# In each attention step, the scalar engine's exponential is issued ahead of the ring's evictions

## The chip, the cores and the metric

The kernel runs on one core of a Trainium2 chip. The time is device time from start to end of one launch, in microseconds (us). The core's engines each run their own instruction list in order and meet only through semaphores: TensorE (PE, with its weight loads shown as PEld), VectorE (DVE), ScalarE (ACT), GpSimd (POOL) and SyncE (SP), which issues the transfers.

## What is computed

Three layers in a row: attention, a mixture of experts, and a gated MLP. The change touches the attention alone, which is this (batch 4, 8 heads, 576 tokens, head size 64):

```python
scores = q @ k.T / sqrt(64)
thresh = max(scores, axis=-1) - tau
scores = where(scores >= thresh, scores, -1e9)
attn = exp(scores - max(scores, axis=-1))
attn = attn / (sum(attn, axis=-1) + 1e-09)
out = attn @ v
```

Its output feeds a router (logits, argmax, a scan over the tokens of a batch, ranks per expert), then the experts and the last layer.

## The kernel before, in words

**Units and steps.** Two heads make a pair; there are 16 pairs. A pair has 9 units (`W = 9`) of 128 rows of scores by 576 columns, the last of them packed from the two heads' last 64 rows. So there are 144 units, and the program is a list of numbered steps, one for each unit and some after them. I write w0 to w8 for the place of a step in its pair, S(w) for the score product of unit w, and "of the pair before" where a step of one pair handles work of the last.

**What each engine does in step n.**

- PE first computes the scores of unit n+1 into one of three score buffers in PSUM (`ps_s`, L556 and L557). It waits there until the mask of unit n-2 is done, since that frees the buffer. Then it fills the items of step n.
- DVE takes the row maximum of unit n (L802), normalises the pv items of step n-1 (L841), masks unit n-1 (L816: keep what is above the floor, times the exponential, with the row sum), and makes the floor of unit n (L807). In w1 it also sums and inverts a whole pair's row sums (L823, L830).
- ACT takes the exponential of unit n (L467; it waits for the row maximum of unit n) and evicts the items of step n that are not DVE's (L510; each waits for its fill). In w2 and w3 it also scales half of the next pair's q (L463). POOL splits q and k into high and low parts for the pair after.

**The ring.** All transposes and products after the scores go through a ring of two PSUM banks, `ps_ring`. Item number i may be filled only when item i-2 has been taken out. The items of a pair, in order of filling, with the step in which they stand:

| step | items filled by PE (line) | taken out by |
|---|---|---|
| w3 to w8, then w0 and w1 of the next pair | main 0 to 7: four transposes of one unit's probabilities (L604) | ACT |
| w2 of the next pair | tails and last: what is left of the transposes (L610, L616) | ACT |
| w4 of the next pair, ahead of its main item | sums and rest (L620 to L626) | ACT |
| w5, w7 of the next pair, w0, w2 of the one after | pv 0 to 3: 20 products of transposed probabilities and v (L635), last in their step | DVE |

So w2 holds tails, last, pv 3, and pv 3 can start only when tails has been evicted; in w4, main 1 can start only when sums has been evicted. In pairs 5 to 7, 9 to 11 and 13 to 15 some steps hold a router item more (logits, rows, spread), and w1 of pairs 8 and 12 holds two. The router item rows 3 stands in w6 behind main 3, and can be filled only when DVE has taken pv 0 of step w5 out. The scan over a batch's tokens (L898) stands on DVE at the end of w5 of pairs 7, 11 and 15.

Nothing plans the order: it is what the step loops of the functions say. Here they are, with the lines that the change touches:

Of the kernel before, what the change touches and what calls it, by code (L numbers as in the profile page):

```python
# [52 lines left out]
def rows(t):  # L53
    return P if t < FULL else TAIL
# [10 lines left out]
UNITS = ALL_PAIRS * W  # L65
# [18 lines left out]
def after_batch(b, at):  # L84

    return PAIRS * W * (b + 1) + at
# [60 lines left out]
def taken_from_ring(kind, i, of):  # L147

    return taken(filled(kind, i, of))
# [7 lines left out]
def unit_of(n):  # L157

    return divmod(n, W)


def attention(nc, ctx, io, route):
# [127 lines left out]
    def q_head(h, part):  # L290

        return q_split[0][part, (S + TAIL) * h:(S + TAIL) * h + S]

    def scores(n):
        return ps_s[:, n % SLOTS_S, :, 0:HALF]
# [162 lines left out]
    def scalar_steps(act, steps, row_banks=None):  # L458

        def scale_q(pair, h):  # L460

            act.wait_ge(q_loaded, 32 * pair + 32)
            nc.scalar.mul(q_in[:, h, :], q_in[:, h, :], float(DH) ** -0.5).then_inc(q_scaled, 1)  # L463

        def exp_scores(n):
            act.wait_ge(maxed, n + 1)
            nc.scalar.activation(expd[:, n % SLOTS_S, :].rearrange("p (a c) -> p a c", a=2), scores(n), ACT.Exp,  # L467
                                 bias=max_tau[:, n % 4, 0:1]).then_inc(exped, 1)

        def evacuate(no, item):  # L470

            kind, i, of = item
            act.wait_ge(turned, no + 1)
            bank = ps_r[:, no % 2, :]
            pt = probs_t[of % 2]
            if kind == "main":
                t, h = divmod(i, 2)
                out, src = pt[:, FULL * h:FULL * h + FULL, P * t:P * t + P], bank.rearrange("p (c q) -> p c q", c=FULL)
            elif kind == "tails":
                out, src = pt[:, W - 1, 0:FULL * P], bank  # L480
            elif kind == "last":
                out = pt[:, 0:2 * FULL, FULL * P:S].rearrange("p (h c) q -> p c h q", h=2)
                src = bank.rearrange("p (c h q) -> p c h q", c=FULL, h=2)
            elif kind == "sums":
                if of >= 2:

                    act.wait_ge(dve_took, taken_from_ring("pv", PIECES - 1, of - 2))
                out, src = pt[:, W, 0:FULL * P], bank
            elif kind == "rest":
                nc.scalar.copy(pt[0:DH, W - 1:W + 1, FULL * P:S], bank[0:DH, 0:2 * P].rearrange("p (a q) -> p a q", a=2)[:, :, 0:TAIL])  # L490
                out, src = pt[DH:P, W - 1:W + 1, FULL * P:S], bank[DH:P, 0:2 * P].rearrange("p (a q) -> p a q", a=2)[:, :, TAIL:P]
            elif kind == "logits":
                r = rows(i)
                out, src = logits[0:r, i, :], bank[0:r, 0:E + 1]
            elif kind == "early":
                nc.scalar.copy(logits[0:TAIL, FULL, :], bank[0:TAIL, FULL * (E + 1):QT * (E + 1)])
                out, src = logits[:, 0:FULL, :], bank[:, 0:FULL * (E + 1)].rearrange("p (t e) -> p t e", t=FULL)
            elif kind == "rows":
                if i == 0 and of > 0:

                    act.wait_ge(rows_stored, 32 * of)
                r = rows(i)
                out, src = x_rows[0:r, i, :], bank[0:r, 0:D]
            elif kind == "spread":
                cols = FULL * P if i == 0 else TAIL
                out, src = code_r[:, FULL * P * i:FULL * P * i + cols], bank[0:E, 0:cols]
            else:
                nc.scalar.copy(onehot_t[0:TAIL, FULL, :], bank[0:TAIL, FULL * E:QT * E])
                out, src = onehot_t[:, 0:FULL, :], bank[:, 0:FULL * E].rearrange("p (t e) -> p t e", t=FULL)
            nc.scalar.copy(out, src).then_inc(evacuated, 1)  # L510

        def last_rows(i):

            act.wait_ge(rows_turned, i + 1)
            if i == 0:

                act.wait_ge(rows_stored, 32 * (B - 1))
            r = rows(i)
            nc.scalar.copy(x_rows[0:r, i, :], row_banks[i][0:r, :]).then_inc(rows_out, 1)

        def exp_logits(b):
            act.wait_ge(shift_done, b + 1)
            nc.scalar.activation(exp_l[:], shifted[:], ACT.Exp).then_inc(exp_done, 1)

        if steps.start == 0:
            for h in range(2):
                act.wait_ge(q_loaded if h else q_first, 32)
                nc.scalar.mul(q_in[:, h, :], q_in[:, h, :], float(DH) ** -0.5).then_inc(first_scaled, 1)
                act.wait_ge(first_scaled, h + 1)
                nc.scalar.copy(q_head(h, slice(0, P)), q_in[:, h, :]).then_inc(first_cast, 1)  # L530

        for n in steps:
            pair, w = unit_of(n)
            for k, item in enumerate(STEPS[n]):
                if item[0] not in BY_DVE:
                    evacuate(FIRST_OF_STEP[n] + k, item)
            if n < UNITS:
                exp_scores(n)
            for h in range(2):
                if w == SCALE_AT[h] and pair + 1 < ALL_PAIRS:  # L540
                    scale_q(pair + 1, h)
            for b in range(B):
                if n == after_batch(b, ARGMAX_AT + 1 if b < B - 1 else LAST_ARGMAX_AT):
                    exp_logits(b)
            for i in range(QT):
                if n == after_batch(B - 1, LAST_ROWS_AT[i]):
                    last_rows(i)

    @block.scalar
    def _(act):  # L550
        scalar_steps(act, range(MAIN_STEPS))
# [468 lines left out]
    def _(dve):  # L1020
# [4 lines left out]
    left = range(MAIN_STEPS, len(STEPS))  # L1025
    return Ending(
        sync=lambda sp: store_rows(sp, B - 1), scalar=lambda act, row_banks: scalar_steps(act, left, row_banks),
        tensor=lambda pe, row_banks: tensor_steps(pe, left, row_banks), vector=lambda dve: vector_steps(dve, left),
        probs=lambda dve: vector_steps(dve, range(len(STEPS), len(STEPS) + 1)), rows_stored=rows_stored, slots_known=slots_known,
# [747 lines left out]
```

## Time and profile before

| | |
|---|---|
| median of three runs | 981.18 us (978.01 to 984.55) |
| profiled execution | 986.12 us, of which the span is 984.3 us |
| attention | from the start to about 376 us of the span |
| PE busy | 907.7 us, 92% of the span |
| DVE busy | 552.4 us, 56% |
| ACT busy | 416.1 us, 42% |
| POOL busy | 381.5 us, 39% |

The profiled execution is 4.9 us above the median. PE is the busiest engine over the whole span. In the attention stage the other engines are busy too: the page's slices show PE at 8 or 9 tenths, DVE at 7 and ACT at 6 through the first eleven of 40 slices. How to read a time line: start, length, engine, line, what it writes from what it reads, how many instructions are merged, and in brackets how long the engine stood idle before it and which instruction ended that. A length includes an end that overlaps the next instruction: a copy of 0.59 us on ACT is followed by the next instruction 0.48 us after its start.

### The profile page before, as it was taken

What the parts mean: (1) busy time and instruction counts of PE and PEld (TensorE: products, weight loads), DVE (VectorE), ACT (ScalarE), POOL (GpSimd) and SP (SyncE); (2) the same over time, 40 slices, a digit from 0 to 9 for tenths busy, and PEclk for the clock granted to TensorE, in tenths of its full rate; (3) what the DMA queues carried; (4) which work ended last, traced back from release to release, by engine and by line L of the source; (5) the groups of instructions that cost most, each with busy time, mean ns of one, the idle gap of its engine ahead of it and who ended that gap; (6) DMA issues with size and microseconds to landing.
All of it is one profiled execution on the core that took longest, in us unless ns stands there. A gap on an engine that the chain in (4) does not pass through costs nothing.

```text
span 984.3 us, 16278 instructions
## 1 busy us (share of the span) xinstructions
PE 907.7 (92%) x6007; PEld 766.9 (78%) x6007; DVE 552.4 (56%) x1206; ACT 416.1 (42%) x794; POOL 381.5 (39%) x347
## 2 busy tenths in 40 slices
PE   6899998999889993999999999999879999999996
PEld 5777887788778782788888888788669788798885
DVE  6777777777777726705846578460034435344351
ACT  4766666666666623233333333333323122131220
POOL 4344435644473133345655556554204013040100
PEclk8999999999999986899999999999979999999998
DMA  5323322232232016423656376430030020200101
GB/s 147 74 61 87 83 74 61 62 110 62 72 109 63 13 49 232 157 89 122 214 162 196 129 220 200 154 101 19 0 109 1 1 97 1 83 14 1 49 1 49
DMA packets 47709, 86.82 MB, mean 88 GB/s; under 512 B 8076, under 2 KB 16396, under 8 KB 47632
## 3 DMA queue, kind: packets, MB, share of 16 engines
q1 hardware_dynamic: 43632, 76.32, 25.9%
q0 software_dynamic: 4000, 9.45, 3.0%
q8 instruction: 51, 0.84, 0.4%
q14 instruction: 26, 0.21, 0.1%
HBM read 73.42 MB, written 15.99 MB: 91 GB/s over the span
## 4 chain that ended last, share of the span: by engine, by line
PE 51%; DVE 6%; DMA 4%; issue 1%; ACT 1%; POOL 0%; DVEq 0%; POOLq 0%
PE ps_h L1357 4%; PE ps_h L1359 4%; PE ps_h L1358 4%; PE ps_y L1376 4%; PE ps_y L1378 4%; PE ps_y L1377 4%; PE ps_a L1639 4%; PE ps_a L1640 4%; PE ps_a L1641 4%; PE ps_v L1639 3%; DMA w_raw<-in_w 3%; PE ps_v L1641 2%; PE ps_v L1640 2%; PE ps_r L1639 2%; PE ps_r L1640 2%; PE ps_r L1641 2%
## 5 line engine op out<-in xcount | busy, mean ns | idle before, releaser
L816 DVE SCALAR_TENSOR_TENSOR probs<-ps_s,floor,expd 128x576 f32<-128x576 f32 x144 | 117.1, 813 | 62.0 <-ACT expd L467 61.6
L510 ACT COPY probs_t<-ps_ring 128x512 f32<-128x512 f32 (+1 forms) x192 | 105.9, 560 | 102.5 <-PE ps_ring L604 93.4
L1289 DVE CAST w_high<-w_raw 128x1024 fp32r<-128x1024 f32 (+1 forms) x63 | 66.8, 1076 | 103.6 <-PE ps_h L1359 52.1
L556 PE MATMUL ps_s<-k_high,q_split 128*128 128x288 f32 x336 | 107.0, 336 | 15.1 <-DVE probs L816 11.1
L467 ACT ACTIVATE expd<-ps_s,max_tau 128x576 f32<-128x576 f32 x144 | 108.0, 750 | 4.8 <-DVE max_tau L802 4.7
L802 DVE TENSOR_REDUCE max_tau<-ps_s 128x1 f32<-128x576 f32 x144 | 106.8, 742 | 0.0
L635 PE MATMUL ps_ring<-probs_t,v_pair 128*64 128x144 f32 x1280 | 94.8, 296 | 3.6 <-ACT probs_t L510 3.6
L556 PEld LDWEIGHTS ps_s<-k_high,q_split 128*128 128x128 f32 x336 | 64.6, 192 | 36.4 <-DVE probs L816 25.3
L557 PE MATMUL ps_s<-k_low,q_split 128*128 128x288 f32 x336 | 92.6, 298 | 0.0
L635 PEld LDWEIGHTS ps_ring<-probs_t,v_pair 128*64 128x64 f32 x1280 | 78.2, 140 | 14.7 <-ACT probs_t L510 7.1
L604 PE MATMUL ps_ring<-ident,probs 128*128 128x128 f32 x512 | 80.0, 279 | 8.0 <-ACT probs_t L510 8.0
L1516 POOL TENSOR_TENSOR rstd<-var_eps,exponent 128x1 f32<-128x1 f32 (+1 forms) x20 | 17.0, 849 | 180.7 <-DVE var_eps L1578 180.7
L1357 PE MATMUL ps_h<-w_high,x_slot_t_high 128*128 x200 | 82.8, 414 | 4.4 <-POOL x_slot_t_low L1179 2.4
L1376 PE MATMUL ps_y<-w_high,hidden_t_high 128*128 128x512 f32 x200 | 80.9, 405 | 2.3 <-DVE w_low L1297 1.9
L1297 DVE TENSOR_TENSOR w_low<-w_raw,w_high 128x1024 fp32r<-128x1024 f32 x66 | 80.8, 1246 | 0.0
L1359 PE MATMUL ps_h<-w_high,x_slot_t_low 128*128 x200 | 79.7, 398 | 0.0
L1358 PE MATMUL ps_h<-w_low,x_slot_t_high 128*128 x200 | 79.4, 397 | 0.0
L1378 PE MATMUL ps_y<-w_high,hidden_t_low 128*128 128x512 f32 x200 | 78.4, 392 | 0.0
L1377 PE MATMUL ps_y<-w_low,hidden_t_high 128*128 128x512 f32 x200 | 77.9, 390 | 0.0
L1191 POOL DMA_INDIRECT y_rows_dram<-scratch,ids x25 | 32.6, 1303 | 113.6 <-ACT scratch L1240 113.6
L604 PEld LDWEIGHTS ps_ring<-ident,probs 128*128 128x128 f32 x512 | 61.3, 142 | 12.2 <-ACT probs_t L510 11.4
L1229 ACT ACTIVATE scratch<-ps_h 128x512 f32<-128x512 f32 x50 | 29.9, 599 | 90.3 <-PE ps_h L1359 84.9
(238 smaller groups left out, 2058.5 us busy)
## 6 DMA issues: line engine op xcount, KB each, us to landing
w_raw<-in_w SPq DMA_DIRECT2D x64, 512.0 KB
k_in<-in_k SPq DMA_DIRECT2D x30, 288.0 KB, 4.2
q_in<-in_q SPq DMA_DIRECT2D x30, 288.0 KB, 4.2
v_pair<-in_v SPq DMA_DIRECT2D x16, 256.0 KB, 2.7
x_rows_dram<-scratch SPq DMA_DIRECT2D x4, 1024.0 KB, 4.6
out<-scratch SPq DMA_DIRECT2D x4, 1024.0 KB, 4.3
scratch<-in_dense SPq DMA_DIRECT2D x8, 384.0 KB, 6.1
scratch<-y_rows_dram SPq DMA_DIRECT2D x3, 1024.0 KB, 5.5
```

The costliest lines, as they stand in the source:

```text
L467: nc.scalar.activation(expd[:, n % SLOTS_S, :].rearrange("p (a c) -> p a c", a=2), scores(n), ACT.Exp, bias=max_tau[:, n % 4, 0:1]).then_i ...
L556: nc.tensor.matmul(out, lhs, k_high[par][:, h, cols], start=first, stop=False)
L604: last = nc.tensor.transpose(bank[:, P * c:P * c + P], src[:, at + P * c:at + P * c + P], ident[:])
L635: last = nc.tensor.matmul(bank[DH * h:DH * h + DH, 0:PIECE], v[:, c, DH * h:DH * h + DH], pt[:, chunk, cols], start=(c == 0), stop=(c == Q ...
L802: nc.vector.tensor_reduce(max_tau[:, n % 4, 0:1], scores(n), AX_XY, ALU.max, negate=True).then_inc(maxed, 1)
L816: nc.vector.scalar_tensor_tensor(out=row_of(pair, w).rearrange("p (a c) -> p a c", a=2), in0=scores(n), scalar=floor[:, n % 4:n % 4 + 1], ...
L1357: nc.tensor.matmul(ps_h[:, half, :], x_slot_t[0][:, c, :], high[:, cols], start=(c == 0), stop=False)
L1358: nc.tensor.matmul(ps_h[:, half, :], x_slot_t[0][:, c, :], low[:, cols], start=False, stop=False)
L1359: last = nc.tensor.matmul(ps_h[:, half, :], x_slot_t[1][:, c, :], high[:, cols], start=False, stop=(c == DC - 1))
L1376: nc.tensor.matmul(ps_y[:], hidden_t[0][:, c, :], high[:, cols], start=(c == 0), stop=False)
L1377: nc.tensor.matmul(ps_y[:], hidden_t[0][:, c, :], low[:, cols], start=False, stop=False)
L1378: last = nc.tensor.matmul(ps_y[:], hidden_t[1][:, c, :], high[:, cols], start=False, stop=(c == FC - 1))
```

## The change

In every step ACT now issues the exponential ahead of the evictions of the same step. No instruction is added or removed, none changes its form, and only ACT's list is reordered.

```diff
         for n in steps:
             pair, w = unit_of(n)
+            if n < UNITS:
+                exp_scores(n)
             for k, item in enumerate(STEPS[n]):
                 if item[0] not in BY_DVE:
                     evacuate(FIRST_OF_STEP[n] + k, item)
-            if n < UNITS:
-                exp_scores(n)
             for h in range(2):
                 if w == SCALE_AT[h] and pair + 1 < ALL_PAIRS:
                     scale_q(pair + 1, h)
```

ACT, steps w2, w3 and w4 of pair 2, before. `turned` is the count of filled ring items, `maxed` that of row maxima. The two copies at the top are tails and last, the third main 0, then sums, rest in two parts, and main 1.

```order
L510 COPY probs_t<-ps_ring 128x512 [waits turned]
L510 COPY probs_t<-ps_ring 128x4x2x64 [waits turned]
L467 ACTIVATE expd<-ps_s,max_tau 128x576 [waits maxed]
L463 ACTIVATE q_in<-q_in 128x576 [waits q_loaded]
L510 COPY probs_t<-ps_ring 128x4x128 [waits turned]
L467 ACTIVATE expd<-ps_s,max_tau 128x576 [waits maxed]
L463 ACTIVATE q_in<-q_in 128x576 [waits q_loaded]
L510 COPY probs_t<-ps_ring 128x512 [waits turned]
L490 COPY probs_t<-ps_ring 64x2x64 [waits turned]
L510 COPY probs_t<-ps_ring 64x2x64
L510 COPY probs_t<-ps_ring 128x4x128 [waits turned]
L467 ACTIVATE expd<-ps_s,max_tau 128x576 [waits maxed]
```

The same three steps with the change:

```order
L467 ACTIVATE expd<-ps_s,max_tau 128x576 [waits maxed]
L510 COPY probs_t<-ps_ring 128x512 [waits turned]
L510 COPY probs_t<-ps_ring 128x4x2x64 [waits turned]
L463 ACTIVATE q_in<-q_in 128x576 [waits q_loaded]
L467 ACTIVATE expd<-ps_s,max_tau 128x576 [waits maxed]
L510 COPY probs_t<-ps_ring 128x4x128 [waits turned]
L463 ACTIVATE q_in<-q_in 128x576 [waits q_loaded]
L467 ACTIVATE expd<-ps_s,max_tau 128x576 [waits maxed]
L510 COPY probs_t<-ps_ring 128x512 [waits turned]
L490 COPY probs_t<-ps_ring 64x2x64 [waits turned]
L510 COPY probs_t<-ps_ring 64x2x64
L510 COPY probs_t<-ps_ring 128x4x128 [waits turned]
```

Each exponential has moved up past its own step's copies: past tails and last in w2, past main 0 in w3, and past four copies in w4. The scaling of q stays where it was.

ACT at the end of w4 and in w5 and w6 of pair 2, before (main 1, exponential of w4, main 2, exponential of w5, main 3, exponential of w6):

```order
59 L510 COPY probs_t0<-ps_ring 128x4x128 [waits turned]
60 L467 ACTIVATE expd<-ps_s,max_tau 128x576 [waits maxed]
61 L510 COPY probs_t0<-ps_ring 128x4x128 [waits turned]
62 L467 ACTIVATE expd<-ps_s,max_tau 128x576 [waits maxed]
63 L510 COPY probs_t0<-ps_ring 128x4x128 [waits turned]
64 L467 ACTIVATE expd<-ps_s,max_tau 128x576 [waits maxed]
```

and with the change (main 1, exponential of w5, main 2, exponential of w6, main 3):

```order
60 L510 COPY probs_t0<-ps_ring 128x4x128 [waits turned]
61 L467 ACTIVATE expd<-ps_s,max_tau 128x576 [waits maxed]
62 L510 COPY probs_t0<-ps_ring 128x4x128 [waits turned]
63 L467 ACTIVATE expd<-ps_s,max_tau 128x576 [waits maxed]
64 L510 COPY probs_t0<-ps_ring 128x4x128 [waits turned]
```

The exponential of w4 is gone from between main 1 and main 2, since it now stands ahead of sums; otherwise copies and exponentials alternate as before, each exponential one copy earlier.

## Rows read from the trace of the kernel before

**Rows 1.** Waits, 16 to 345 us: who waited for whom, us, times, longest

```profile
ACT probs_t L510 <- PE ps_ring L604: 91.5, 93, 1.6
DVE probs L816 <- ACT expd L467: 60.4, 67, 2.6
```

**Rows 2.** Time line of PE, pairs 3 and 4, without router items

```profile
79.00 1.45 PE L635 MATMUL ps_ring<-probs_t,v_pair 128*64 128x144 f32 x20
...
81.97 0.40 PE L556 MATMUL ps_s<-k_high,q_split 128*128 128x288 f32 x1 [0.36 <-DVE probs L816]
...
83.81 1.45 PE L635 MATMUL ps_ring<-probs_t,v_pair 128*64 128x144 f32 x20
...
86.40 0.40 PE L556 MATMUL ps_s<-k_high,q_split 128*128 128x288 f32 x1
...
87.56 1.45 PE L635 MATMUL ps_ring<-probs_t,v_pair 128*64 128x144 f32 x20
...
92.20 1.45 PE L635 MATMUL ps_ring<-probs_t,v_pair 128*64 128x144 f32 x20 [0.24 <-ACT probs_t L510]
...
97.18 0.66 PE L604 MATMUL ps_ring<-ident,probs 128*128 128x128 f32 x4 [0.67 <-ACT probs_t L510]
```

**Rows 3.** Time line of ACT in the same stretch, w2 to w4

```profile
91.56 1.07 ACT L510 COPY probs_t<-ps_ring 128x512 f32<-128x512 f32 x2
...
95.33 0.75 ACT L467 ACTIVATE expd<-ps_s,max_tau 128x576 f32<-128x576 f32 x1
95.97 0.68 ACT L463 ACTIVATE q_in<-q_in 128x576 f32<-128x576 f32 x1
96.54 0.59 ACT L510 COPY probs_t<-ps_ring 128x512 f32<-128x512 f32 x1
```

**Rows 4.** Time line of DVE in the same stretch

```profile
79.41 0.82 DVE L816 SCALAR_TENSOR_TENSOR probs<-ps_s,floor,expd 128x576 f32<-128x576 f32 x1 [1.47 <-ACT expd L467]
...
85.31 0.31 DVE L841 TENSOR_TENSOR x_t<-ps_ring,probs_t 128x144 f32<-128x144 f32 x1 [0.84 <-PE ps_ring L635]
85.53 0.81 DVE L816 SCALAR_TENSOR_TENSOR probs<-ps_s,floor,expd 128x576 f32<-128x576 f32 x1
...
89.42 0.81 DVE L816 SCALAR_TENSOR_TENSOR probs<-ps_s,floor,expd 128x576 f32<-128x576 f32 x1
...
90.55 0.70 DVE L802 TENSOR_REDUCE max_tau<-ps_s 128x1 f32<-128x576 f32 x1
```

**Rows 5.** Time line of DVE, the first units and the mask of unit 3

```profile
10.84 0.76 DVE L802 TENSOR_REDUCE max_tau<-ps_s 128x1 f32<-128x576 f32 x1
...
13.88 0.81 DVE L816 SCALAR_TENSOR_TENSOR probs<-ps_s,floor,expd 128x576 f32<-128x576 f32 x1
...
15.34 0.81 DVE L816 SCALAR_TENSOR_TENSOR probs<-ps_s,floor,expd 128x576 f32<-128x576 f32 x1
...
19.51 0.82 DVE L816 SCALAR_TENSOR_TENSOR probs<-ps_s,floor,expd 128x576 f32<-128x576 f32 x1 [2.61 <-ACT expd L467]
```

**Rows 6.** Time line of ACT, the first exponentials

```profile
11.63 1.60 ACT L467 ACTIVATE expd<-ps_s,max_tau 128x576 f32<-128x576 f32 x2 [2.84 <-DVE max_tau L802]
```

**Rows 7.** Time line of PE, the first pv product (pair 1, w5)

```profile
39.54 1.45 PE L635 MATMUL ps_ring<-probs_t,v_pair 128*64 128x144 f32 x20
```

**Rows 8.** Windows: us, busy PE, PEld, DVE, ACT, POOL, PEclk, DMA share, GB/s

```profile
22.00:26.00 4.00, 3.92 (x19) 3.81 (x20) 2.91 (x9) 2.12 (x4) 1.98 (x1) 0.57 0.37 72
```

**Rows 9.** Time line of PE, w5 to w7 of pair 7

```profile
162.24 1.45 PE L635 MATMUL ps_ring<-probs_t,v_pair 128*64 128x144 f32 x20
...
166.22 0.66 PE L660 MATMUL ps_ring<-ident,x_t 128*128 128x128 f32 x4 [1.38 <-DVE scratch L841]
...
168.81 1.45 PE L635 MATMUL ps_ring<-probs_t,v_pair 128*64 128x144 f32 x20
```

**Rows 10.** Time line of DVE, end of w4 and w5 of pair 7

```profile
162.64 0.82 DVE L816 SCALAR_TENSOR_TENSOR probs<-ps_s,floor,expd 128x576 f32<-128x576 f32 x1 [1.47 <-ACT expd L467]
...
163.45 1.85 DVE L898 TENSOR_TENSOR_SCAN scratch<-scratch 8x576 f32<-8x576 f32 x1
```

## The prediction

> **What bounds the kernel now.** I read the waits first. ACT waits 91.5 us for transposes in the ring, and DVE waits 60.4 us for the exponential before its masks [rows 1]. So ACT sits waiting for a ring item while the exponential that DVE needs is queued behind that item's copy. Whether this costs anything is a question for PE, which is the busiest engine. So I went to the time lines of one plain pair (without router items), and looked at which of PE's starts has a wait in front of it. I use the four pv products as marks, since each is followed by fixed work. From pv 0 to pv 1 it is 4.81 us, from pv 1 to pv 2 3.75, from pv 2 to pv 3 4.64 [rows 2]. PE stands still at three kinds of places: at S(w8), for a mask; at pv 3, for the copy of tails; at main 1, for the copy of sums [rows 2].
>
> **The shortest chain behind a pv product.** DVE takes a pv item in order, so it holds up the next mask. Where DVE was idle already, the item is taken 1.50 us after the product's start (83.81 to 85.31), the mask starts 0.22 later (85.53), and the score product that needs its buffer 0.87 after that (86.40) [rows 2, 4]. That is 2.59 us, and no order on ACT shortens it. The stretch from pv 1 to pv 2 is on this chain now (83.81 to 86.40 is 2.59), so it stays at 3.75.
>
> **Term A, S(w8): faster.** S(w8) needs the mask of w5, which DVE reaches late, because the mask of w4 before it waited 1.47 us for its exponential [rows 4]. That exponential stood behind the copies of sums, rest (two) and main 1. Now it stands ahead of all four, and DVE is back on the shortest chain: pv 0 + 2.59 to S(w8), and 1.84 more to pv 1 (81.97 to 83.81) [rows 2], 4.43 instead of 4.81. It saves 0.38 us where w6 has no router item: pairs 1 to 4, 8 and 12. Six times, 2.3 us. In the others PE's router work fills the gap already.
>
> **Term B, pv 3: slower.** This is what the order takes back. The copy of tails, which pv 3 needs, now stands behind the exponential of w2, and so behind the row maximum of w2, which comes after pv 2 was taken, a mask, and the summing of the pair's rows. The chain: pv 2 to its taking 1.50, 0.22 to the mask, 1.13 from that mask to the maximum of w2 (89.42 to 90.55) [rows 4], 0.79 from a maximum's start to the exponential (10.84 to 11.63) [rows 5, 6], 0.64 until the next ACT instruction (95.33 to 95.97), and 0.64 from a copy's start to the fill that waits for it (91.56 to 92.20) [rows 2, 3]. Sum 4.92, against 4.64 now: 0.28 lost. It bites where w1 has no router item: pairs 2 to 5, 9 and 13. Six times, minus 1.7 us. Its bounds are 0, if PE is late there for a reason of its own, and 1.0 each, if DVE comes to that maximum one more mask (0.73 from 13.88 to the next unit's maximum, half of 1.46 [rows 5]) later than this chain has it.
>
> **Term C, main 1: nothing.** Main 1 waits for the copy of sums. Before it, ACT does main 0's copy, an exponential and a scaling; now the copy, the scaling and the next exponential: the same two instructions, 95.33 to 96.54, 1.21 us, then 0.64 to main 1 [rows 2, 3]. The stall of 0.67 stays.
>
> **Term D, w6 of pairs 7, 11 and 15: faster.** There the scan follows the mask of w4, and rows 3 may only be filled when pv 0 has been taken, after the scan. The mask of w4 again waited 1.47 us, the scan started at 163.45 and took 1.85, and PE stood 1.38 us at rows 3 [rows 9, 10]. With the change the exponential of w4 goes 2.4 us earlier (it starts one exponential, 0.64, ahead of the copy of sums, instead of behind it by 0.64 for the fill of main 1, about as much until main 1's copy, and 0.48 for that copy; 91.56 holds two copies in 1.07, so one costs 0.48 [rows 3]), so the mask starts near 160.2, the scan near 161.0 (0.81 later, as in rows 10), the maximum of w6 at about 162.9, and DVE is free at 163.5, before pv 0 can be taken (162.24 + 1.50 = 163.74). So the 1.38 goes, and the late mask for S(w8) as in term A, 0.38: 1.8 us. I count 1.8, 1.8 and, in pair 15, whose scan is half a us shorter, 1.3: 4.9 us. Bounds: 0 if something else in that step is late too, 5.4 if all of 1.8 comes three times.
>
> **Term E, the start: faster.** Up to the first pv product PE mostly waits for masks. The exponential of unit 3 waited for a transfer of q that ACT scales first; now it goes one copy (0.48) earlier. From the mask of unit 3 (19.51) to pv 0 of pair 1 (39.54) it takes 20.0 us for eleven units, 1.82 each; DVE alone needs 1.46 a unit (13.88 to 15.34) and 0.33 for one pair's sums, 16.4 [rows 5, 7]. Upper bound 0.48 + 3.6 = 4.1. But at 22 to 26 us the granted clock is 0.57, close to the lower of its two levels (1.2 of 2.4 GHz), and PE is busy 3.92 of 4.00 us [rows 8]: there PE itself is the limit, and an earlier mask gives nothing. The lower bound is the one copy skipped, 0.5. I take 2.5, nearer the middle, since the slow stretch is a part of the twenty us.
>
> The Trainium skill (TensorE: Matmul & The Clock Gate, Part 1) says that the throttled state is the default and activity releases it. By that rule fewer waits at the start would bring the full clock sooner, and E would be at its upper end; no row here tells how soon, so the rule is a rival below and not in the sum.
>
> **Sum.** 2.3 - 1.7 + 0 + 4.9 + 2.5 = 8.0 us. The profiled execution of 986.12 us would be 978.1. It lies 4.9 above the median of 981.18, so for the median I forecast 981.2 - 8.0 = 973.2 us, 0.8% faster. Everything behind the attention (experts, last layer) follows PE and moves as a whole, as no instruction there is changed.
>
> About 1% is what a measurement of this kernel can tell from no change, so this forecast lies just inside "the same".
>
> **Rivals.**
>
> - *The start at full clock.* PE waits less, the clock is at its upper level through the first 40 us, E gives 4.1, D 5.4 and B half: 2.3 - 0.9 + 5.4 + 4.1 = 10.9, so 970.3 us. For it: the clock was already at 0.57 with the waits of the old order [rows 8]. Against: DVE at 1.46 us a unit would still set the pace, so PE keeps gaps. Chance 0.2.
> - *The exponential was not what set the end.* Another wait stands right behind each one that goes (the ring, or the mask by way of pv). Then A is as computed, since its chain is read from the rows, but D falls to the 0.38 of S(w8) and E to 0.5: 2.3 - 1.7 + 1.1 + 0.5 = 2.2, so 979.0 us. For it: term C, where exactly this happens. Chance 0.2.
> - *The ring becomes the bound (slower).* Every copy now waits for a row maximum. If DVE comes to the maximum of w2 one mask (0.73) later than I have it, the stall at pv 3 grows by 1.0 us (0.28 + 0.73), and not only in six pairs but in the 15 that have a pv 3, since the delay is longer than what a router item hides: 15 us lost. A DVE that late gives nothing in D; with A at 2.3 and E at 0.5 the median is 981.2 + 15 - 2.8 = 993.4 us. A smaller lateness, 0.5 in each of 15 pairs, gives 986. It decides from about 0.4 us on. Against it: DVE waits 60 us for ACT now [rows 1], and that slack is what it gets back. Chance 0.08, half of it at the smaller size.
> - *The forecast*, 973.2 us with its own range of 970 to 977: chance 0.52.
>
> Faster by over 1% means below 971.4: most of the first rival (0.17) and the fast tail of the forecast (0.13), 0.30. Slower by over 1% (above 991): 0.04. The rest, 0.66, is within 1%. The range reaches from the first rival with a little run-to-run spread, 968, to just beyond the second, 981.
>
> **What would show it in the new profile.** DVE's wait for the exponential drops from 60.4 us to below 10. ACT's wait for a row maximum appears. In a plain pair: 4.4 us from pv 0 to pv 1, 3.75 from pv 1 to pv 2, 4.9 from pv 2 to pv 3, with a longer wait in front of pv 3 for ACT's copy; 0.67 still in front of main 1. No wait of 1.4 us in front of rows 3. First pv product near 37 us. If the pv 2 to pv 3 stretch is 5.5 or more, the ring rival is right; if pv 0 to pv 1 is still 4.8, the exponential was not the cause.

## The result and the profile after

The change gives 971.52 us (median of four runs, 970.18 to 972.48) against 980.86 us for the kernel before on the same chip (978.01 to 984.55). The ratio is 0.9896, with a 95% interval of 0.9869 to 0.9923: about 1% faster. The forecast was 973.2 us, the range 968 to 981. The profiled execution took 972.48 us (span 970.7), against 986.12 (span 984.3) before.

**Waits.** The waits of the changed kernel over the same stretch (who waited for whom, us, times, longest); they answer to [rows 1]:

```profile
ACT probs_t L510 <- PE ps_ring L604: 75.9, 87, 1.6
ACT expd L467 <- DVE max_tau L802: 14.4, 27, 1.5
DVE probs L816 <- ACT expd L467: 2.0, 3, 1.6
```

DVE's wait for the exponential has gone from 60.4 us to 2.0. In its place ACT waits 14.4 us for row maxima, where it was 1.1.

**A plain pair.** PE of pairs 3 and 4, the same stretch as [rows 2]:

```profile
75.70 1.45 PE L635 MATMUL ps_ring<-probs_t,v_pair 128*64 128x144 f32 x20
...
78.30 0.40 PE L556 MATMUL ps_s<-k_high,q_split 128*128 128x288 f32 x1
...
80.14 1.45 PE L635 MATMUL ps_ring<-probs_t,v_pair 128*64 128x144 f32 x20
...
83.90 1.45 PE L635 MATMUL ps_ring<-probs_t,v_pair 128*64 128x144 f32 x20
...
88.74 1.45 PE L635 MATMUL ps_ring<-probs_t,v_pair 128*64 128x144 f32 x20 [0.58 <-ACT probs_t L510]
...
93.72 0.66 PE L604 MATMUL ps_ring<-ident,probs 128*128 128x128 f32 x4 [0.67 <-ACT probs_t L510]
...
95.28 1.45 PE L635 MATMUL ps_ring<-probs_t,v_pair 128*64 128x144 f32 x20
```

From pv 0 to pv 1 it is now 4.44 us (before 4.81), then 3.76 (3.75), 4.84 (4.64) and 6.54 (6.53). The wait in front of S(w8) is gone. The wait in front of pv 3 has grown from 0.24 to 0.58. Main 1 still waits 0.67.

**What stands in front of pv 3 now.** DVE, the mask after pv 2's taking, the sums, and the maximum of w2; and ACT, the exponential of w2 and the two copies behind it (tails is the first):

```profile
85.39 0.31 DVE L841 TENSOR_TENSOR x_t<-ps_ring,probs_t 128x144 f32<-128x144 f32 x1 [0.52 <-PE ps_ring L635]
85.62 0.81 DVE L816 SCALAR_TENSOR_TENSOR probs<-ps_s,floor,expd 128x576 f32<-128x576 f32 x1
...
86.42 0.16 DVE L823 TENSOR_REDUCE row_sum<-sum_eps 128x9 f32<-128x18 f32 x1
86.61 0.22 DVE L830 RECIPROCAL inv_sum<-row_sum 128x9 f32<-128x9 f32 x1
86.74 0.70 DVE L802 TENSOR_REDUCE max_tau<-ps_s 128x1 f32<-128x576 f32 x1
```

```profile
87.47 0.74 ACT L467 ACTIVATE expd<-ps_s,max_tau 128x576 f32<-128x576 f32 x1 [0.34 <-DVE max_tau L802]
88.11 1.06 ACT L510 COPY probs_t<-ps_ring 128x512 f32<-128x512 f32 x2
```

**Pair 7 and the start.** PE in w5 to w7 of pair 7, to be held against [rows 9], and the first pv product of the program [rows 7]; then the clock window of [rows 8]:

```profile
158.69 1.45 PE L635 MATMUL ps_ring<-probs_t,v_pair 128*64 128x144 f32 x20
...
161.13 0.60 PE L660 MATMUL ps_ring<-ident,x_t 128*128 128x128 f32 x4
...
163.31 1.45 PE L635 MATMUL ps_ring<-probs_t,v_pair 128*64 128x144 f32 x20
```

```profile
22.00:26.00 4.00, 3.66 (x29) 3.19 (x27) 4.00 (x13) 3.22 (x6) 1.95 (x1) 1.00 0.44 96
```

Rows 3 has no wait in front of it: 4.62 us from pv 0 to pv 1, where it was 6.57. The first pv product stands at 36.62 instead of 39.54. In this execution the granted clock was 1.00 at 22 to 26 us, before it was 0.57.

**The sum of the attention.** The last of the marks, pv 3 in the second to last pair, stands at 341.80 instead of 351.85: 10.05 us. The start gives 2.92 of it; the six stretches from pv 0 to pv 1 give 6 x 0.37 = 2.2; the three with the scan 1.95 + 1.94 + 1.44 = 5.3; two stretches that the prediction did not have give 1.2 (below); the stretches into pv 3 take back 1.65. Together 10.0. The rest of the 13.6 us between the two spans lies behind these marks, where both kernels have the same instructions. The first window behind the last mark, of the kernel before and of the change (same work, 16.46 and 14.89 us, granted clock 0.79 and 0.89), holds 1.6 us of it:

```profile
351.85:368.31 16.46, 15.83 (x151) 14.57 (x151) 3.71 (x18) 1.74 (x6) 7.16 (x10) 0.79 0.01 1
```

```profile
341.80:356.69 14.89, 14.25 (x151) 12.99 (x151) 3.71 (x18) 1.73 (x6) 7.13 (x10) 0.89 0.01 2
```

About 1 us each lies in the experts and in the last layer. The profiled execution of before lay about 5 us above its median, that of the change 1 us above its own.

### The profile page after: what moved, and what is told of

Its sections match the earlier page's. It is cut to its first block, busy times and chain, and to the rows that moved or that the text cites. A ratio compares the mean times of both kernels' runs of the same rounds, so it can differ in the third digit from the quotient of the medians.

```text
span 970.7 us, 16278 instructions
## 1 busy us (share of the span) xinstructions
PE 902.7 (93%) x6007; PEld 763.5 (79%) x6007; DVE 550.1 (57%) x1206; ACT 417.1 (43%) x794; POOL 384.8 (40%) x347
## 4 chain that ended last, share of the span: by engine, by line
PE 54%; DVE 4%; DMA 2%; issue 1%; ACT 1%; POOL 0%; DVEq 0%; POOLq 0%
PE ps_h L1357 4%; PE ps_h L1359 4%; PE ps_y L1376 4%; PE ps_h L1358 4%; PE ps_y L1378 4%; PE ps_y L1377 4%; PE ps_a L1639 4%; PE ps_a L1641 4%; PE ps_a L1640 4%; PE ps_v L1639 3%; PE ps_v L1641 2%; PE ps_v L1640 2%; PE ps_r L1639 2%; PE ps_r L1640 2%; PE ps_r L1641 2%; PE ps_ht L1341 2%
## 5 line engine op out<-in xcount | busy, mean ns | idle before, releaser
L1289 DVE CAST w_high<-w_raw 128x1024 fp32r<-128x1024 f32 (+1 forms) x63 | 60.4, 975 | 103.5 <-PE ps_h L1359 52.0
L467 ACT ACTIVATE expd<-ps_s,max_tau 128x576 f32<-128x576 f32 x144 | 107.3, 745 | 19.6 <-DVE max_tau L802 18.7
L635 PE MATMUL ps_ring<-probs_t,v_pair 128*64 128x144 f32 x1280 | 93.9, 294 | 5.6 <-ACT probs_t L510 5.6
L635 PEld LDWEIGHTS ps_ring<-probs_t,v_pair 128*64 128x64 f32 x1280 | 77.2, 139 | 16.8 <-ACT probs_t L510 9.1
L1297 DVE TENSOR_TENSOR w_low<-w_raw,w_high 128x1024 fp32r<-128x1024 f32 x66 | 85.4, 1315 | 0.0
```

Of the source, the lines that this page charges most:

```text
L635: last = nc.tensor.matmul(bank[DH * h:DH * h + DH, 0:PIECE], v[:, c, DH * h:DH * h + DH], pt[:, chunk, cols], start=(c == 0), stop=(c == Q ...
```

## The experiments

The kernels of the experiments replace the change's two lines by a condition. Their line numbers are shifted by a few (L635 becomes L638 to L641). All give as marks the stretches pv 0 to 1, 1 to 2, 2 to 3 and 3 to the next 0 in a plain pair; before it is 4.81, 3.75, 4.64, 6.53, with the change 4.44, 3.75, 4.84, 6.52.

```diff
+            ahead = w == 4          # the condition of the experiment
+            if n < UNITS and ahead:
+                exp_scores(n)
             for k, item in enumerate(STEPS[n]):
                 ...
-            if n < UNITS:
+            if n < UNITS and not ahead:
                 exp_scores(n)
```

### Only the exponential of w4 ahead

`ahead = w == 4`.

> The exponential goes ahead of the evictions in step w4 of each pair alone; elsewhere the order is that of before. Theory 1 (the gain comes from single places): the exponential of w4, queued behind four copies, was the cause of terms A and D. So pv 0 to pv 1 is 4.44 us in plain pairs and 4.62 in pairs 7, 11 and 15, as with the whole change, pv 2 to pv 3 stays at 4.64, and the time falls by 2.2 + 5.3 = 7.5 us, plus a few tenths in pair 1. Theory 2 (every earlier exponential helps a little, the gain is spread over the nine steps): about 1 us, and pv 0 to pv 1 stays near 4.8.

Measured: 987.21 us, ratio 1.0055 (1.0028 to 1.0083), slower than before, where I had expected 7.5 us less. The stretches: 4.44, 3.75, 4.62, 7.18. So term A is confirmed as it was reasoned: the late exponential of w4, and it alone, held up S(w8). But the last stretch has grown by 0.65. ACT, w3 and w4, and PE at main 1:

```profile
95.31 0.59 ACT L510 COPY probs_t<-ps_ring 128x512 f32<-128x512 f32 x1 [1.00 <-PE ps_ring L607]
95.80 0.75 ACT L467 ACTIVATE expd<-ps_s,max_tau 128x576 f32<-128x576 f32 x1
96.43 0.68 ACT L463 ACTIVATE q_in<-q_in 128x576 f32<-128x576 f32 x1
97.00 0.74 ACT L467 ACTIVATE expd<-ps_s,max_tau 128x576 f32<-128x576 f32 x1
97.63 0.59 ACT L510 COPY probs_t<-ps_ring 128x512 f32<-128x512 f32 x1
```

```profile
98.28 0.66 PE L607 MATMUL ps_ring<-ident,probs 128*128 128x128 f32 x4 [1.31 <-ACT probs_t L510]
```

Between the copy of main 0 (95.31) and that of sums (97.63) there are now two exponentials and a scaling: the one of w3, which has not moved, and the one of w4, which has. Main 1 waits 1.31 instead of 0.67, in nearly every pair. So a move of one step's exponential is not a part of the whole change: it puts two exponentials into one gap of the ring. In the whole change each gap loses one and gains one, which is term C.

This run showed a second thing, in pair 7: pv 0 to pv 1 was 5.92 there, not the 4.62 that an early mask gives, while in pair 15 it was 4.63. I come to it with the scan.

### Only the exponentials of w3 and w4 ahead

`ahead = w in (3, 4)`. It repairs that gap.

> The exponential goes ahead in steps w3 and w4 alone. Theory 1a (what w4 alone missed: with w3 unmoved, two exponentials stand between main 0's copy and that of sums, 0.64 us more; moving both leaves one): pv 0 to pv 1 4.44, pv 3 to the next pv 0 back at 6.53, 4.62 in pairs 7, 11 and 15, no wait for the ids in pairs 9 and 13. A, D and the ids give 2.2 + 5.3 + 1.2 = 8.7 us, and the start is that of before. Rival (the length of the stretch behind pv 3 is set by something else that w4 alone disturbed, the masks for instance): 7.1 or so stays, and the time is near that of before.

Measured: 973.07 us, ratio 0.9902 (0.9871 to 0.9934). The stretches: 4.43, 3.75, 4.63, 6.53: all the gain of A, none of the loss of B. Terms A, C and D stand on these two steps. DVE's wait for the exponential is still 32.3 us in this kernel, and the marks show no cost of it: the size of a wait on an engine that is not the bottleneck says little.

Here too one gap of the ring holds two exponentials, the one between the copies of last and of main 0 (w2, not moved, and w3). ACT in w2 and w3 of pair 4, the two copies at the top being tails and last:

```profile
89.75 1.08 ACT L510 COPY probs_t<-ps_ring 128x512 f32<-128x512 f32 x2
90.70 0.76 ACT L467 ACTIVATE expd<-ps_s,max_tau 128x576 f32<-128x576 f32 x1
91.34 0.69 ACT L463 ACTIVATE q_in<-q_in 128x576 f32<-128x576 f32 x1
91.91 0.76 ACT L467 ACTIVATE expd<-ps_s,max_tau 128x576 f32<-128x576 f32 x1
93.03 0.59 ACT L510 COPY probs_t<-ps_ring 128x512 f32<-128x512 f32 x1 [0.36 <-PE ps_ring L607]
```

It costs nothing: ACT still waits 0.36 us for main 0 to be filled, since pv 3 stands on PE in between. A full gap costs where PE is waiting at its end.

### Only the exponential of w2 ahead

`ahead = w == 2`.

> The exponential goes ahead in step w2 alone. Theory 1: the loss by itself: pv 2 to pv 3 4.84 in plain pairs, pv 0 to pv 1 unchanged at 4.81; 1 to 2 us slower than before. Theory 2: about 1 us faster than before. In pair 0 (no ring items in w2) nothing changes.

Measured: 985.62 us, ratio 1.0037 (1.0010 to 1.0064). The stretches: 4.81, 3.76, 5.04, 6.53. Here too two exponentials (w1, not moved, and w2) stand between the copies of main 7 and of tails, so pv 2 to pv 3 is 0.4 longer than before, more than the 0.2 of the whole change, and router pairs lose as well (6.34 became 6.84 from pair 6 into 7, and from 10 into 11). It has the sign of term B, costs more than the 1 to 2 us expected, and shows again that single moves don't add up.

### All but w2

`ahead = w != 2`.

> The change in all steps but w2, where tails and last are evicted first, as before. Theory 1: only the loss of term B goes. pv 2 to pv 3 is 4.64 instead of 4.84 in plain pairs and 5.3 instead of 5.6 in pair 9 and 13, all else as with the change: 1.6 us faster than the change, about 11.5 us faster than before. Theory 2: w2 was one of nine steps that helped, so it is about 1 us slower than the change.

Measured: 970.94 us, ratio 0.9897 (0.9865 to 0.9929). The stretches: 4.44, 3.75, 4.50, 6.54. Pv 2 to pv 3 has fallen from 4.84 to 4.50, below the 4.64 of before that I had expected: between the copies of main 7 and of tails there stood one exponential before (w1), one with the change (w2), and here there is none. So term B is the exponential of w2 ahead of tails. Over the six places that is 2 us less than the change, too little for the total to show beside its spread, and the profiled execution began its pairs 1.4 us later (38.03).

### Only the first 14 steps

`ahead = n < 14`.

> The exponential goes ahead only in steps 0 to 13 (pair 0, and pair 1 up to w4). Theory 1: term E by itself: the first pv product near 36.6 us of the span instead of 39.5, all later pairs as before, 2.5 to 3 us faster than before. If the gain at the start was the granted clock and not the order (rival: in the profile of before it was 0.57 at 22 to 26 us, in that of the change 1.00), then it shows only in executions with the clock high there, and here the first pv product comes at 38 us or later where the clock in 22 to 26 us is low.

Measured: 979.24 us, ratio 0.9966 (0.9934 to 0.9998). The first pv product stands at 36.67, as in the change, pair 1 has 4.45 from pv 0 to pv 1 (before 4.80), and all stretches up to the last mark behind that are those of before. So the start is worth 2.9 us by itself in this execution (clock 1.00 at 22 to 26 us), with 0.4 in pair 1, and the total of 3.3 (982.50 less 979.24) agrees.

### The start: order or clock?

The change was run two more times, beside other kernels.

> The change itself once more, on the same chip and beside the same runs as the three kernels below. About 1.0% faster than before. If the granted clock at 22 to 26 us is a draw of the run and not a consequence of the order, the first pv product comes either at 36.6 us (clock 1.00) or at about 38.0 us (clock near 0.6) with the same order.

> The change once more, beside the three others on the same chip: 970 to 972 us, ratio 0.989. Every theory gives the same; it is the comparison for the other three. The first pv product shows again whether its place follows the granted clock at 22 to 26 us: 36.6 with 1.00, 37.8 with 0.70.

Measured: 970.61 us, ratio 0.9890 (0.9847 to 0.9932), and 973.54 us, ratio 0.9895 (0.9864 to 0.9926). The windows from 22 to 26 us of the two:

```profile
22.00:26.00 4.00, 4.00 (x24) 3.83 (x24) 3.45 (x12) 2.81 (x5) 2.55 (x1) 0.70 0.44 105
```

```profile
22.00:26.00 4.00, 3.64 (x30) 3.16 (x28) 4.00 (x13) 3.24 (x6) 1.89 (x1) 1.00 0.37 82
```

With 0.70 the first pv product stands at 37.79, with 1.00 at 36.55: 1.2 us between two executions of the same program. I had expected the clock to make this difference, and it makes half of it. ACT's scaling of q, which the exponential of unit 3 stands behind, waits for a transfer, and that landed 0.6 to 0.7 us later in the execution with 0.70. The first of these lines is from the second run of the change, the other from the third:

```profile
18.24 0.68 ACT L463 ACTIVATE q_in<-q_in 128x576 f32<-128x576 f32 x1 [3.12 <-DMA q_in<-in_q]
17.56 0.69 ACT L463 ACTIVATE q_in<-q_in 128x576 f32<-128x576 f32 x1 [2.78 <-DMA q_in<-in_q]
```

So I count from that scaling to the first pv product. In the three executions with this start and a clock of 1.00 (the change, its third run, the first 14 steps) it is 18.99 us each time, with 0.70 it is 19.55, and in the kernel before, with 0.57, it is 21.87 (17.67 to 39.54). So I put 0.56 us down to the lower clock; all of it lies between the masks of unit 3 and unit 7 (6.73 us against 6.17), from 19.6 to 26.3 us. The order gives 2.3 with the clock low in both (0.57 and 0.70, so a little of it may still be clock) and 2.9 where the change had it at 1.00. That the clock does not do it alone is shown by the kernel with w3 and w4, which had 1.00 in that window too and took 21.12 us, 0.75 less than before, with a part of the order moved. Whether the order makes the full clock more likely is not shown: the windows of before, of w4 alone, of w2 alone and of all but w2 have 0.57 to 0.61, but each is one execution.

### The sums out of the chain to pv 3

The change, with DVE's sums and reciprocals of a pair moved to the step after:

```diff
-            if w == 1 and 0 < pair <= ALL_PAIRS:
+            if w == 2 and 0 < pair <= ALL_PAIRS:
                 add_eps(pair - 1)
```

> The change, with DVE's summing and inverting of a pair's row sums moved from w1 to w2 (behind the mask of that step). Theory of term B: in the changed kernel pv 3 waits for a chain that runs from the taking of pv 2 by way of a mask, the sums, the row maximum of w2 and its exponential to the copy of tails; the two small sum instructions stand 0.33 us long in that chain (87.60 to 87.93 in the repeated run of the change). Out of it, the exponential can start 0.27 us earlier (0.33 less the 0.06 by which a maximum behind the sums is shorter): pv 2 to pv 3 goes from 4.85 to 4.58 in the plain pairs and from 5.64 to about 5.37 in pairs 8 and 12, all else as in the change: about 1.6 to 2 us less in all, a ratio near 0.987 to the kernel before. Rival: the copy of tails waits for its transposes on PE or for ACT's work ahead of it, and not for that maximum: 4.85 stays and the time is the change's (970.6). Second rival: the sums in w2 hold up DVE there, so that main 0 or sums come late, and pv 3 to pv 0 grows beyond 6.52: 1 to 3 us slower than the change.

Measured: 969.04 us, ratio 0.9857 (0.9825 to 0.9889); its six runs (965.93 to 970.97) lie below all six of the change on the same chip (971.96 to 974.37). The stretches: 4.44, 3.76, 4.57, 6.54. DVE and ACT in front of pv 3:

```profile
85.43 0.75 DVE L805 TENSOR_REDUCE max_tau<-ps_s 128x1 f32<-128x576 f32 x1
...
86.90 0.16 DVE L826 TENSOR_REDUCE row_sum<-sum_eps 128x9 f32<-128x18 f32 x1
```

```profile
86.21 0.74 ACT L467 ACTIVATE expd<-ps_s,max_tau 128x576 f32<-128x576 f32 x1
86.85 1.06 ACT L510 COPY probs_t<-ps_ring 128x512 f32<-128x512 f32 x2
```

The exponential still starts 0.03 us behind the end of its maximum, but both come earlier: from pv 2 to this exponential it is 3.30 us (82.91 to 86.21), where the change has 3.57 (83.90 to 87.47). That is the 0.27 computed, and pv 2 to pv 3 is 4.57 (4.58 computed); the two stretches from pairs 8 and 12 into the pairs after are 5.36 and 5.34 (5.37 expected). Over the six that is 1.7 us, the place of the last mark less its start (303.61 against 305.27) agrees. So the two links of term B's chain that a move can take out, the exponential of w2 and the sums, are shown by runs; the others are read from the rows. The other 2 to 3 us by which the total is lower lie behind the attention or at the start, and I have no experiment on them.

### The scalings of q elsewhere

The stall at main 1 has a scaling of q in front of it. Here the scalings stand in w0 and w1 instead of w2 and w3, from pair 1 on, with the change and with the change but for w2.

```diff
-                if w == SCALE_AT[h] and pair + 1 < ALL_PAIRS:
+                if w == (SCALE_AT[h] if pair == 0 else (0, 1)[h]) and pair + 1 < ALL_PAIRS:
```

> The change, and from pair 1 on the two halves of q are scaled in w0 and w1 instead of w2 and w3. Theory (term C: the 0.67 us at main 1 is ACT's queue, main 0's copy, a scaling and an exponential in a row): with the scaling gone the copy of sums starts when sums is filled or the exponential of w4 is done, 0.45 us earlier, so 0.2 of the wait at main 1 is left and pv 3 to the next pv 0 is 6.1 instead of 6.53. In 15 pairs 6.5 us faster than the change, about 16 us faster than before. Rival (main 1 waits because the maximum of w4 is late, not for the queue): no more than 0.1 us a pair, 1 us in all. A third way: the scaling in w1 delays the copy of tails, and pv 2 to pv 3 grows above 4.84.

> The same, and in w2 the evictions of tails and last stay ahead of the exponential. Theory: pv 2 to pv 3 is 4.50 and pv 3 to the next pv 0 6.1 in plain pairs, 2 us less than with the scaling early alone and 8 us less than the change: about 18 us faster than before, ratio 0.982. Rival: the exponential of w2 now stands right ahead of the one of w3 and main 0's copy, and delays that copy; then what is won at pv 3 is lost at main 1.

Measured: 973.73 us, ratio 0.9911 (0.9886 to 0.9936), no better than the change, where I had expected 6.5 us less; and 966.0 us, ratio 0.9863 (0.9797 to 0.9929), where I had expected 0.982. The four runs of the second reach from 962.83 to 976.22, so its total can't be told from the change's, but its last mark stands at 337.38, against 342.98 in the second run of the change. Main 1's stall fell to 0.26 and the last stretch to 6.13 in both. In the first the gain was lost elsewhere. The scaling of w1 stands ahead of the exponential of w2, so tails comes later (4.97 instead of 4.84, and 7.19 instead of 6.40 from pair 6 into 7 and from 10 into 11, where the second kernel has 6.74). And in pairs 7 and 11 pv 0 to pv 1 was 5.99 and 5.96 instead of 4.63. The first I had named as a third way, the second not. The second is the scan.

### The scan and GpSimd

Before, the scan took 1.85 us in pairs 7 and 11 [rows 10] and 1.33 in pair 15. In the change it takes 1.33 in all three; with the early scalings 3.48 in pairs 7 and 11, with w4 alone 3.41. DVE's scan and GpSimd's subtraction for the next pair's q: in pair 7 of the kernel before (the scan is in [rows 10]), of w4 alone, of the early scalings, and of the third run of the change:

```profile
161.46 2.64 POOL L404 TENSOR_TENSOR q_split<-q_in,q_split 64x1152 fp32r<-64x1152 f32 x1
```

```profile
163.45 2.64 POOL L404 TENSOR_TENSOR q_split<-q_in,q_split 64x1152 fp32r<-64x1152 f32 x1
163.90 3.41 DVE L901 TENSOR_TENSOR_SCAN scratch<-scratch 8x576 f32<-8x576 f32 x1
```

```profile
156.42 2.65 POOL L405 TENSOR_TENSOR q_split<-q_in,q_split 64x1152 fp32r<-64x1152 f32 x1
156.79 3.48 DVE L902 TENSOR_TENSOR_SCAN scratch<-scratch 8x576 f32<-8x576 f32 x1
```

```profile
157.44 1.33 DVE L898 TENSOR_TENSOR_SCAN scratch<-scratch 8x576 f32<-8x576 f32 x1
157.57 3.65 POOL L404 TENSOR_TENSOR q_split<-q_in,q_split 64x1152 fp32r<-64x1152 f32 x1
```

Where the subtraction starts first, the scan ends 1.20 to 1.22 us after the subtraction's end (164.10 and 165.30; 166.09 and 167.31; 159.07 and 160.27), however early the scan was issued. Where the scan starts first, the subtraction is 1.0 us longer. In the kernel with the sums moved it was another instruction of GpSimd, the copy ahead of the subtraction, that began 0.03 us behind the scan of pair 7, and it took 2.26 us instead of 1.14. The test lets the subtraction wait, in the kernel with the early scalings:

```diff
+            if pair in (8, 12):
+                pool.wait_ge(chosen, (pair - 4) // 4)
             nc.gpsimd.tensor_tensor(low, q_in[DH:P, :, :], low.bitcast(F32), ALU.subtract)
```

> The kernel with the early scaling of q (scale_early), in which GpSimd's subtraction for pairs 8 and 12 waits until VectorE's scan over the batch is done. In scale_early the subtraction had started 0.37 us ahead of the scan, and the scan took 3.48 us instead of 1.33 and ended 1.20 us after the subtraction; in the kernel before it was 1.85 us with the subtraction 1.99 us ahead (end again 1.20 after it); in the change, where the scan starts first, 1.33 us, and the subtraction is 1.0 us longer. Theory: the two can't run side by side, and whichever starts first holds the other up. Then both scans take 1.33 us here, and the stretch from pv 0 to pv 1 of pairs 7 and 11 goes from 5.99 and 5.96 back to 4.63: 2.7 us less than scale_early's 973.7, so about 971.0, no more than the change's time again. Rival: the scan's length is set by something else in that step (the matrix engine's rows, its own operands): 3.48 stays and nothing is gained. Second rival: scans become short, but the late split of q holds up the score products of the next pair, and w8 or w0 after it grows by up to 1 us: no gain in all.

Measured: 971.75 us, ratio 0.9875 (0.9842 to 0.9908). GpSimd and DVE of pair 7:

```profile
157.35 1.33 DVE L904 TENSOR_TENSOR_SCAN scratch<-scratch 8x576 f32<-8x576 f32 x1
```

```profile
158.84 2.65 POOL L407 TENSOR_TENSOR q_split<-q_in,q_split 64x1152 fp32r<-64x1152 f32 x1 [1.94 <-DVE scratch L904]
```

Both scans are 1.33 us, and pv 0 to pv 1 is 4.62 in pairs 7 and 11, as expected; nothing behind them became longer. The stretches show 2.7 us of gain; the two kernels' totals were measured on different chips. That one of the two engines stands while the other works is shown. The Trainium skill (SBUF — State Buffer, "SBUF: two separate sides") states it as an exclusive lock on a port pair that the two share, taken for a whole instruction by whichever starts first, where DVE's instruction has two inputs in SBUF and GpSimd's reads SBUF; the scan in pairs 7 and 11 has two, and the numbers above agree. The scan in pair 15 has the same two, but there is no next q to split and so no subtraction beside it: 1.33 or 1.34 in every kernel. What a scan with an input elsewhere does beside GpSimd, no run here shows.

### Put together

All but w2 ahead, the scalings in w0 and w1, the subtraction behind the scan.

> The exponential ahead in every step but w2, q scaled in w0 and w1 of each pair but the first instead of w2 and w3, and GpSimd's subtraction for pairs 8 and 12 behind the scan. Its parts measured so far: pv 2 to pv 3 at 4.51 instead of 4.85 where the exponential of w2 stays behind tails; pv 3 to pv 0 at 6.13 instead of 6.52, since without the scaling in w3 main 1's stall falls from 0.67 to 0.26. Over 14 pairs that is 0.34 x 6 and 0.4 x 8 and smaller gains in router pairs: 5.6 us to the last pv 3 (337.38 against 342.98). The scans were short there by 0.1 us of luck; the wait for them only keeps them so. Expected: 4 to 6 us less than the change on the same chip, a ratio to the kernel before of 0.983 to 0.985. Rival: the wait gives nothing and these gains are taken back by the clock of the last stages: within 1 us of the change.

Measured: 967.63 us, ratio 0.9841 (0.9807 to 0.9876), 6 us below the change on the same chip; its six runs (964.07 to 969.90) lie below all six of the change. The stretches: 4.43, 3.76, 4.50, 6.13. Main 1 and pv 3 in pair 4:

```profile
87.72 1.45 PE L641 MATMUL ps_ring<-probs_t,v_pair 128*64 128x144 f32 x20 [0.24 <-ACT probs_t L513]
...
92.30 0.66 PE L610 MATMUL ps_ring<-ident,probs 128*128 128x128 f32 x4 [0.26 <-ACT probs_t L513]
```

The last mark stands at 337.18, against 341.82, although the start was 0.9 later. This version beats both kernels. The one with the sums moved is near to it (969.04); the two were not tried together.

## Why the prediction was right, point by point

**The shortest chain** behind a pv product held: pv 0 at 75.70 to S(w8) at 78.30 is 2.60, computed 2.59. Every stretch on it is where it was put.

**Term A** (+2.3): 4.81 became 4.44, six times 0.37, 2.2. Shown to be the exponential of w4 by the run with w4 alone.

**Term B** (-1.7): the chain was right and its end 0.08 too late, 4.84 instead of 4.92. The link from the maximum to the exponential is 0.73, not 0.79, since a maximum that follows the short sums is 0.70 long instead of 0.76. In the two places with other work in w2 (from pair 8 to 9 and 12 to 13) it lost 0.30, and some hundredths in router pairs, so the term came to 1.65 all the same. The bounds held.

**Term C** (0): 0.67 before, 0.67 after. The runs with w4 alone (1.31, one exponential more) and with the early scalings (0.26, the scaling gone) show that it follows what stands between main 0's copy and that of sums.

**Term D** (+4.9): 5.3 measured. The scan ended in time and the 1.38 went in pairs 7 and 11, as did the 0.86 in pair 15. Each of the three gave 0.14 us more than counted. The stall of 1.38 is idle time behind the end of main 3, and that end overlaps the next instruction: from main 3 to rows 3 it was 1.98 us (164.24 to 166.22) and is 0.44 (160.69 to 161.13), 1.54 less. I had also taken 1.85 us for the scan, and it is 1.33 when it starts ahead of GpSimd's subtraction, here by 0.12 us; this made no difference to the sum, since DVE would have been free before pv 0 could be taken with 1.85 too (157.43 + 1.85 + 0.70 for the maximum is 159.98, the taking is at 160.18). Half a us is the whole difference between pairs 7 and 11 (1.95, 1.94) and pair 15 (1.44), as counted. I had seen that the last scan was shorter and not asked why. An exponential a few tenths later would have put the scan behind the subtraction's start, and two thirds of the gain in these pairs would have gone, as in the kernel with w4 alone (5.92 instead of 4.62). The prediction had no such case: its rivals for D were a late something, without a place.

**Term E** (+2.5): 2.9 in the profiled execution, and 2.3 with the clock at 0.70, if the transfer of q lands at the same time. The one copy skipped is there: from the scaling of q to the mask of unit 3 it was 1.84 us (17.67 to 19.51), and it is 1.35 (17.63 to 18.98). The rest was a choice inside wide bounds (0.5 to 4.1), so that it came near is in part luck, and its reason (the slow stretch is PE's own) was right for one kind of execution only. The clock of that stretch was read as a property of the kernel, but executions of one and the same kernel differ in it.

**A term that was not there** (+1.2). In w4 of pairs 9 and 13, the item rest waited 0.64 us for DVE to take an item called ids (of w3) out, before: DVE did that behind a mask whose exponential it waited for (a part of the 60.4 us of [rows 1]). PE and DVE in the kernel before:

```profile
204.28 0.33 PE L624 MATMUL ps_ring<-ident,inv_cols 128*128 128x128 f32 x1 [0.64 <-DVE table L946]
```

```profile
203.12 0.82 DVE L816 SCALAR_TENSOR_TENSOR probs<-ps_s,floor,expd 128x576 f32<-128x576 f32 x1 [0.65 <-ACT expd L467]
203.86 0.08 DVE L816 DVE_READ_ACCUMULATOR probs<-ps_s,floor,expd 128x1 f32 x1
203.93 0.30 DVE L946 TENSOR_TENSOR table<-ps_ring,table 128x144 f32<-128x144 f32 x1
```

With the change pv 3 to pv 0 there is 6.66 instead of 7.27, twice 0.6. It is the exponential of w3 that does it: with w4 alone the wait of 0.64 is still there and the stretch is 7.26, with w3 and w4 the wait is gone and it is 6.67. I had gone through the plain pairs and the pairs with a scan, but not through the pairs with ids.

**The sum.** Forecast 8.0 us; the terms in the trace come to 10.0. Of the difference, the missed term is 1.2, D 0.4 (the overlap in the stall that was read) and E 0.4; with the lower clock at the start E would have been 0.2 short instead. The medians differ by 9.3. The mechanism of A to D was right and the sizes nearly so; what the sum lacked was the term of the ids.

**The rivals.** *Start at full clock*: it happened in three of the four executions with the change's start (36.62, 36.55 and 36.67 against 37.79), but gave 2.9 and not 4.1. DVE set the pace, as the counter-argument had it: in the window at 22 to 26 us of the change it is busy 4.00 of 4.00 us and PE 3.66. The rule of the Trainium skill beside it (TensorE: Matmul & The Clock Gate, Part 1), that activity releases the throttled clock, is neither borne out nor refuted by this: one and the same order had 0.70 and 1.00 in that window. *The exponential was not what set the end*: refuted, A and D came in full. *The ring becomes the bound*: refuted for this change, pv 2 to pv 3 is 4.84 and not 5.5 or more. But its mechanism is real where a move is made alone: the runs with w4 or w2 alone are slower than the kernel before by it.

## What to carry to other kernels

When two kinds of work alternate on an in-order engine, count for each gap of the ring how many of the other kind stand in it, before and after; a move in all steps leaves the counts, and a move in one step puts two into one gap. That cost 0.4 to 0.65 us per pair here where PE waited at the end of the gap, and nothing where a pv product stood in it. Ask of every instruction whose length differs from place to place (1.33, 1.85) what else ran beside it; it can be a cost that your change will shift. And take the clock of a short stretch from more than one execution before a term rests on it; where two executions differ, look first for a transfer that landed later.

## What was not expected of the hardware

A scan of 8 x 576 on DVE took 1.33 us alone and up to 3.48 beside a GpSimd subtraction of 64 x 1152 that had started 0.37 us earlier, and it ended 1.2 us after the subtraction each time. The granted clock at 22 to 26 us was 0.70 in one execution and 1.00 in two others of the same program, worth 0.56 us up to the first pv product, about as much as the transfer of q that landed later in the same execution.
